# Means of the values of batch 1: eight keys to a row, added on GpSimd, one product on TensorE

## What is computed

```python
B, H, S, D = 2, 8, 768, 64                     # q, k, v are (B, H, S, D), f32
block, window = 32, 16
nb = S // block                                # 24 blocks
k_sum = k.reshape(B, H, nb, block, D).max(axis=3)
v_sum = v.reshape(B, H, nb, block, D).mean(axis=3)
scores_l = q @ k.T / sqrt(D), kept where |pos_q - pos_k| < window
scores_s = q @ k_sum.T / sqrt(D) + log(block)
a = softmax([scores_l, scores_s])              # over both together
attn = a @ [v, v_sum]
x = attn as (B*S, H*D) = (1536, 512)
x = elu(x @ w_in) @ w_out                      # w_in 512x2048, w_out 2048x512
out = gate * (relu(x @ w1[e]) @ w2[e])         # e, gate: best of 8 experts by cosine, per token
```

## Time and profile before

| | |
|---|---|
| three runs | 546.84, 546.86, 547.81 us |
| profiled execution | 546.45 us (span 544.7 us) |
| TensorE (PE) busy | 532.5 us, 98% of the span |
| TensorE weight loads (PEld) | 458.7 us, beside the products |
| VectorE (DVE), ScalarE (ACT), GpSimd (POOL) busy | 301.7, 234.0, 82.0 us |
| granted TensorE clock, mean | 0.998 |

### The profile page before, as it was taken

One profiled execution on the slowest core, in us unless ns is written; L12 is line 12 of the kernel. 1 busy time (PEld: TensorE's weight loads), 2 busy tenths in 40 slices (PEclk: granted clock), 3 DMA queues, 4 the chain that ended last, 5 costly groups with the idle time before them and its releaser, 6 DMA issues.

```text
span 544.7 us, 11801 instructions
## 1 busy us (share of the span) xinstructions
PE 532.5 (98%) x3930; PEld 458.7 (84%) x3931; DVE 301.7 (55%) x667; ACT 234.0 (43%) x530; POOL 82.0 (15%) x210
## 2 busy tenths in 40 slices
PE   8799999999999999999999999999999999999995
PEld 7688888888888888888889898888788888888883
DVE  3789887544644464447542557667583274322552
ACT  5677764443544453444332436461171251211440
POOL 6312020011100000000000000110312131111221
PEclk9999999999999999999999999999999999999999
DMA  9999322232121112110100720010875155101000
GB/s 208 275 273 315 91 48 64 54 75 71 50 64 24 25 25 64 25 25 15 40 1 2 266 84 0 20 59 2 309 256 185 44 206 188 39 28 35 19 19 24
DMA packets 63499, 49.23 MB, mean 90 GB/s; under 512 B 46038, under 2 KB 52182, under 8 KB 63456
## 3 DMA queue, kind: packets, MB, share of 16 engines
q1 hardware_dynamic: 61056, 42.36, 27.1%
q0 software_dynamic: 2400, 6.30, 3.5%
HBM read 43.40 MB, written 6.82 MB: 92 GB/s over the span
## 4 chain that ended last, share of the span: by engine, by line
PE 97%; ACT 1%; issue 1%; DVE 0%; POOLq 0%; DVEq 0%; ACTq 0%
PE bank L976 25%; PE bank L1020 8%; PE bank L1027 8%; PE bank L1033 8%; PE bank L1188 5%; PE bank L1234 5%; PE bank L1242 5%; PE bank L1196 5%; PE bank L1190 5%; PE bank L1236 5%; PE bank L954 3%; PE bank L936 2%; PE bank L927 2%; PE bank L1226 2%; PE bank L1086 1%; PE bank L832 1%
## 5 line engine op out<-in xcount | busy, mean ns | idle before, releaser
L1395 ACT ACTIVATE el<-bank 128x512 f32<-128x512 f32 x48 | 28.7, 597 | 106.0 <-PE bank L976 105.7
L1700 DVE TENSOR_SCALAR el<-el 128x512 f32<-128x512 f32 x48 | 20.7, 431 | 87.8 <-ACT el L1395 87.8
L976 PE MATMUL bank<-x_hi,w_hi_parts 128*128 128x256 f32 x376 | 60.9, 283 | 0.0
L976 PE MATMUL bank<-x_hi,w_lo_parts 128*128 128x256 f32 x376 | 60.4, 282 | 0.0
L976 PE MATMUL bank<-x_lo,w_hi_parts 128*128 128x256 f32 x376 | 60.2, 282 | 0.0
L976 PEld LDWEIGHTS bank<-x_hi,w_hi_parts 128*128 128x128 f32 x376 | 53.6, 188 | 3.2 <-issue 0.2
L1020 PE MATMUL bank<-w_hi_parts,g_hi 128*128 128x512 f32 x192 | 54.9, 408 | 0.0
L1027 PE MATMUL bank<-w_lo_parts,g_hi 128*128 128x512 f32 x192 | 52.8, 397 | 0.0
L1033 PE MATMUL bank<-w_hi_parts,g_lo 128*128 128x512 f32 x192 | 52.5, 395 | 0.0
L976 PEld LDWEIGHTS bank<-x_lo,w_hi_parts 128*128 128x128 f32 x376 | 51.5, 189 | 0.0
L976 PEld LDWEIGHTS bank<-x_hi,w_lo_parts 128*128 128x128 f32 x376 | 51.3, 188 | 0.0
(11 more groups left out here) (282 smaller groups left out, 917.6 us busy)
## 6 DMA issues: line engine op xcount, KB each, us to landing
raw<-in_moe_w SPq DMA_DIRECT2D x8, 2048.0 KB, 8.9
w_raw<-in_moe_w_in SPq DMA_DIRECT2D x8, 512.0 KB, 7.4
w_raw<-in_moe_w_out SPq DMA_DIRECT2D x8, 512.0 KB, 7.6
k_raw<-in_k SPq DMA_DIRECT2D x16, 192.0 KB, 3.2
v_raw<-in_v SPq DMA_DIRECT2D x8, 384.0 KB, 4.3
x_rows<-x SPq DMA_DIRECT2D x6, 512.0 KB, 4.1
q_raw<-in_q SPq DMA_DIRECT2D x44, 64.0 KB, 2.9
vwin<-in_v SPq DMA_DIRECT2D x32, 72.0 KB, 2.8
```

What stands on the lines that cost most here:

```text
L976: mm = pe.matmul(o, r32(w[:, at:at + P]), r32(x[i % 2][:, c, :]), start=(part == "hh" and c == 0), stop=(part == "lh" and c == DC - 1))
L1395: act.activation(el[n % 2], bank[:, H_BANK[n % 2], :], ACT.Exp).then_inc(e_act, 1)
```

## The change

The values of a pair of batch 1 come with eight keys to a partition, on 96 partitions (2048 bytes for each head). GpSimd adds the eight in three additions: four to four, two to two, one to one (512, 256 and 128 elements on each of 96 partitions), each waiting for the one before. TensorE makes one product for the pair, with a new matrix `mean_rows` (96x24) in place of three with `mean`. GpSimd makes `mean_rows` in `means_of_rows`, a memset and two selects of 24 columns, between `constants` and `key_columns(6)`; `means(g)` has one wait more for it (`rows_ok`). `v_raw1` grows from 768 to 1024 columns; `mean`, which only batch 0 still needs, now lies in it ahead of the first load, and `tab` moves from a buffer of its own into scratch space of the attention's zone.

```diff
+    EIGHT = 8
+    V_ROWS = S // EIGHT
...
-        tab = sb("tab", [1, 5, NSTORE], I32)
...
-            {"k_raw1": [P, S], "v_raw1": [P, S], "q_raw0": [P, TB], "q_raw1": [P, TB],
+            {"k_raw1": [P, S], "v_raw1": [P, 2 * EIGHT * D], "q_raw0": [P, TB], "q_raw1": [P, TB],
...
-             "pT": [P, 4 * P], "qT0": [P, TB], "qT1": [P, TB], "mean": [P, KT, NSUM]},
+             "pT": [P, 4 * P], "qT0": [P, TB], "qT1": [P, TB], "mean_rows": [P, NSUM]},
...
+        mean = v_raw1[:, 0:KT * NSUM].rearrange("p (t n) -> p t n", t=KT)
...
+        tab = scratch(1, 5, NSTORE).bitcast(I32)
...
             def load_v1(g):
                 if g > 0:
                     sp.wait_ge(m_mm, PAIRS + g)
-                load_values(H + 2 * g, v_raw1, ld_v1)
+                head = H + 2 * g
+                sp.dma_start(v_raw1[0:V_ROWS, :].rearrange("p (h n) -> p h n", h=2),
+                             vh[head:head + 2].rearrange("h (p t) d -> p h (t d)", p=V_ROWS)).then_inc(ld_v1, 16)
...
+            def means_of_rows():
+                chain(pool.memset(mean_rows[:, :], 1.0 / BLK))
+                chain(pool.affine_select(out=mean_rows, in_=mean_rows, compare_op=ALU.is_ge, fill=0.0, base=0,
+                                         pattern=[[-BLK, NSUM]], channel_multiplier=EIGHT))
+                chain(pool.affine_select(out=mean_rows, in_=mean_rows, compare_op=ALU.is_ge, fill=0.0, base=BLK - 1,
+                                         pattern=[[BLK, NSUM]], channel_multiplier=-EIGHT))
+                pool.sem_inc(rows_ok, 1)
...
             constants()
+            means_of_rows()
             key_columns(6)
...
-            def add_pairs(g):
-
+            def add_eight(g):
+
+                rows = v_raw1[0:V_ROWS, :].rearrange("p (h t d) -> p h t d", h=2, d=D)
                 pool.wait_ge(ld_v1, 16 * g + 16)
-                two = v_raw1.rearrange("p (h t two d) -> p h t two d", h=2, two=2, d=D)
-                pool.tensor_tensor(two[:, :, :, 0, :], two[:, :, :, 0, :], two[:, :, :, 1, :], ALU.add
-                                   ).then_inc(v_two, 1)
+                for n in (4, 2):
+                    chain(pool.tensor_tensor(rows[:, :, 0:n, :], rows[:, :, 0:n, :], rows[:, :, n:2 * n, :], ALU.add))
+                pool.tensor_tensor(rows[:, :, 0, :], rows[:, :, 0, :], rows[:, :, 1, :], ALU.add).then_inc(v_sum, 1)
...
             def means(g):
-                pe.wait_ge(v_two, g + 1)
+                pe.wait_ge(rows_ok, 1)
+                pe.wait_ge(v_sum, g + 1)
                 pe.wait_ge(vs_ev, PAIRS + g)
                 pe.wait_ge(stt, sum(s_at(u) < M_PLACES[g] for u in UNIT_RANGE if u >= PAIRS))
-                src = v_raw1.rearrange("p (h t d) -> p h t d", h=2, d=D)
-                for t in range(0, KT, 2):
-                    mm = pe.matmul(bank[KW:KC, S_BANK[0], 0:P], mean[:, t, :], src[:, :, t, :],
-                                   start=(t == 0), stop=(t == KT - 2))
+                rows = v_raw1[0:V_ROWS, :].rearrange("p (h t d) -> p h t d", h=2, d=D)
+                mm = pe.matmul(bank[KW:KC, S_BANK[0], 0:P], mean_rows[0:V_ROWS, :], rows[:, :, 0, :],
+                               start=True, stop=True)
                 mm.then_inc(m_mm, 1)
```

More of the change, by code:

```diff
@@ L261, in build @@
         W_HI = W_HI[:, :]
-        (k_raw1, v_raw1, q_raw0, q_raw1, vwin, kT, kb0, kb1, kmaxT, mask, pr0, pr1, pT, qT0, qT1, mean,
+        (k_raw1, v_raw1, q_raw0, q_raw1, vwin, kT, kb0, kb1, kmaxT, mask, pr0, pr1, pT, qT0, qT1, mean_rows,
          raw, c_sb, iota_m) = zone(
             "att",
-            {"k_raw1": [P, S], "v_raw1": [P, S], "q_raw0": [P, TB], "q_raw1": [P, TB],
+            {"k_raw1": [P, S], "v_raw1": [P, 2 * EIGHT * D], "q_raw0": [P, TB], "q_raw1": [P, TB],
              "vwin": [P, PAIRS, WINS, P], "kT": [P, PAIRS, KPAD], "kb0": [P, WINS, KC], "kb1": [P, WINS, KC],
              "kmaxT": [P, PAIRS, NSUM], "mask": [P, 3, KC], "pr0": [P, 4, KC], "pr1": [P, 4, KC],
-             "pT": [P, 4 * P], "qT0": [P, TB], "qT1": [P, TB], "mean": [P, KT, NSUM]},
+             "pT": [P, 4 * P], "qT0": [P, TB], "qT1": [P, TB], "mean_rows": [P, NSUM]},
             {"raw": [P, WSZ], "c_sb": [P, 1536], "iota_m": [P, P]})
+        mean = v_raw1[:, 0:KT * NSUM].rearrange("p (t n) -> p t n", t=KT)
         q_raw, qT, kb = (q_raw0, q_raw1), (qT0, qT1), (kb0, kb1)
@@ L342, in build @@
         ld_win, ld_wout = (sems(" ".join(f"{a}_{s}" for s in range(STEPS))) for a in ("ld_win", "ld_wout"))
-        vw_zero, ident_ok, pads_ok, mean_ok, mask_ok, const_ok, iota_ok, xs_zero = sems(
-            "vw_zero ident_ok pads_ok mean_ok mask_ok const_ok iota_ok xs_zero")
+        vw_zero, ident_ok, pads_ok, mean_ok, rows_ok, mask_ok, const_ok, iota_ok, xs_zero = sems(
+            "vw_zero ident_ok pads_ok mean_ok rows_ok mask_ok const_ok iota_ok xs_zero")
         dve_c, pool_c, passed = sems("dve_c pool_c passed")
-        k_t, k_ev, kmx, kb_ev, q_t, q_ev, v_two, m_mm, vs_ev = sems(
-            "k_t k_ev kmx kb_ev q_t q_ev v_two m_mm vs_ev")
+        k_t, k_ev, kmx, kb_ev, q_t, q_ev, v_sum, m_mm, vs_ev = sems(
+            "k_t k_ev kmx kb_ev q_t q_ev v_sum m_mm vs_ev")
         s_mm, mask_h, mask_l, unit_ok, stt, smax, expd, rden_v, rinv_v, norm_v, p_t, pT_ev, o_mm, xh_ev, xl_ev = sems(
@@ L730, in _ @@
             key_columns(8)
-            def add_pairs(g):
+            def add_eight(g):
+                rows = v_raw1[0:V_ROWS, :].rearrange("p (h t d) -> p h t d", h=2, d=D)
                 pool.wait_ge(ld_v1, 16 * g + 16)
-                two = v_raw1.rearrange("p (h t two d) -> p h t two d", h=2, two=2, d=D)
-                pool.tensor_tensor(two[:, :, :, 0, :], two[:, :, :, 0, :], two[:, :, :, 1, :], ALU.add
-                                   ).then_inc(v_two, 1)
+                for n in (4, 2):
+                    chain(pool.tensor_tensor(rows[:, :, 0:n, :], rows[:, :, 0:n, :], rows[:, :, n:2 * n, :], ALU.add))
+                pool.tensor_tensor(rows[:, :, 0, :], rows[:, :, 0, :], rows[:, :, 1, :], ALU.add).then_inc(v_sum, 1)
             for u in range(9, UNITS):
                 if 0 <= u - 3 * PAIRS < PAIRS:
-                    add_pairs(u - 3 * PAIRS)
+                    add_eight(u - 3 * PAIRS)
                 key_columns(u)
```

## The result

The changed kernel takes 542.39 us (median of four runs, 542.21 to 543.25) against 547.3 us before (546.84 to 547.81): ratio 0.9908, 95% interval [0.9896, 0.9921]. The profiled execution took 542.21 us, with a span of 540.5 us.

A forecast was written before the change was run, and what follows sets the result against it. TensorE, busy 98% of the span, was taken to bound the kernel. Sixteen records fewer save 1.76 us, all other terms count as nothing: 546.86 - 1.76 = 545.1 us, range 544.5 to 546.7 us.

The forecast's parts named there:

- What bounds the kernel: TensorE, busy 98% of the span, sets the end; time taken off its queue comes off the end.
- the three waits behind 160 us: TensorE's waits after all four means, 0.4 to 0.6 us each, 1.3 us together, expected to move with TensorE.
- What is removed on TensorE: At batch 1's means, four records fewer per pair at 0.11 us: 0.44 us a pair, 1.76 us for four.
- the 0.12 us of the change of shape and the idle 0.20 us: Part of each means piece that stays, ending with the weight side idle for 0.20 us behind the means.
- The cheap record of batch 0: Rival price from batch 0's means: 0.060 us a record, 0.95 us saved, 545.9 us; chance of its family 0.18.
- the 55.6 ns of the Trainium skill: Rival price from the skill's page for successive 128-column products: 16 records at 55.6 ns, 0.89 us saved.
- The wait for `rows_ok`: One wait more per pair in TensorE's queue at the means: taken at nothing, at most 0.8 us in all.
- What is added to GpSimd: A pair's additions take 2.5 us, bounds 1.93 and 3.03, so 1.5 us more, all off the path.
- the cover: Slack hiding longer GpSimd additions: sums over 8 us early; delayed VectorE instructions end by 81.8 us, read from 83.21.
- The profiled execution and the median: The median of three runs was put 0.41 us above the profiled execution, giving 546.86 us before the change.
- Buffers: Large buffers slide by 560 bytes, those behind by 16; an address was taken to have no price.
- Rivals: Records worth less, 0.18; gain taken back behind, 0.09; GpSimd late, 0.05; change not doing what it says, part of 0.09.

The follow-up runs named there:

- e9: The changed kernel with the weights 32 bytes lower and the buffers of x, g and h 32 bytes higher; 535.91 us.
- e7: The changed kernel with two 32-byte buffers allocated behind the attention's zone, so that the weights begin at 21440; 535.98 us, ratio 0.9789.
- e10: The kernel before, its work untouched, with the weights 64 bytes lower and the buffers of x, g and h 32 bytes higher; 536.32 us, ratio 0.9797.
- e1: The kernel before again, unchanged, for a second trace; 547.75 us.
- e5: The kernel before with `tab` moved into scratch space and 32 bytes left free, weights at 21504 as in the changed kernel; 543.68 us, ratio 0.9935.
- e3: The changed kernel with `gate_cur` allocated behind the attention's zone, so that the weights begin 32 bytes lower; 544.45 us, ratio 0.9942.
- e8: The changed kernel with the buffers of x, g and h 64 bytes higher and the weights where they are; 533.92 us, ratio 0.9753.

## Why the prediction was right and wrong

- **What bounds the kernel:** right. The 1.75 us and the unforeseen gains of TensorE reached the end, but for e9 and e7, where later loads ahead of the means took up most of the 1.75 us (0.4 and 0.3 us left against e10). One reading was off: the shortest of the three waits behind 160 us is 0.3 us, not 0.4; their sum of 1.3 us holds.
- **What is removed on TensorE:** right. 0.44 us for a pair forecast, 0.435 to 0.444 measured; the 0.12 us of the change of shape and the idle 0.20 us stayed. The cheap record of batch 0 (0.060 us, 0.95 us in all) and the 55.6 ns of the Trainium skill (TensorE: Matmul & The Clock Gate, "Wait — 56ns, not 53.3ns?"; 0.89 us, measured with bf16) both fail as prices of these f32 records by the steps: a removed record gave back 0.11 us. The 96 partitions cost nothing.
- **The wait for `rows_ok`:** costs nothing that the 0.33 us piece would show.
- **What is added to GpSimd:** 2.6 us for a pair (2.09 + 0.46) where 2.5 was taken, and the sums stood at 116.5 us for a product at 124.95, 8.5 us early (8.7 forecast). The first pair's took 3.8 us, beyond the 3.0 us of the bound, since VectorE was busy beside it; its two instructions there took 1.03 and 1.75 us in place of 0.69 and 1.22. VectorE's two ended at 80.4 us, and their readers start at 82.71 us and later, so the cover held. The contention that the Trainium skill names (GPSIMD Engine Reference, "1. Specifications") is in this trace; its rule against additions on GpSimd ("4.1 Engine selection") would have misled on the time.
- **The profiled execution and the median:** wrong by a little. The median had been put 0.41 us above the profiled execution; over 17 runs beside the first experiments it was 547.5 us, 1.05 us above. The profiled execution lacked part of the early waits that e1 shows, 1.1 us by 60 us. The changed kernel's profiled execution lies only 0.18 us below its median. Its loads of `w_in` land sooner (5.9 in place of 7.4 us); that this is why is not shown.
- **Buffers:** this is the step that failed. It said that the buffers slide and that "an address has no price that the trace could show", on the ground of three forms of L976 with 283, 282 and 282 ns. Twice wrong. The duration of a record holds its way through the array and hides 1 or 2 ns of pace: the same three forms have 284, 282 and 282 ns in the changed kernel. The distance between starts, or the length of 24 in the chain, shows it. And the three forms could not have told: `w_hi_parts` and `w_lo_parts` lie 65536 bytes apart, `x_hi0` and `x_lo0` 4096, and each tile within them starts a multiple of 512 bytes further. All of them have one and the same distance up to a multiple of 512. The comparison held the disputed quantity fixed. The slide itself was mis-sized too: 480 bytes in place of 560, and 64 bytes up in place of 16 down for the buffers behind. Measured in e5, the moved `tab` and the slid buffers are worth 3.8 us, over twice the work that the change is named for.
- **Rivals:** none of the four happened. Unnamed costs of moved buffers were put on the slower side alone; they were a gain, and twice the size of the forecast.

The forecast direction was right for its reason, and the size was wrong for a cause that the change carries along. That this cause helped and did not hurt was luck: the forecast had no term for it, and other slides of 32 or 64 bytes made the changed kernel 2.1 us slower (e3) or 6 to 8 us faster (e7, e8). A line that moves a table of 480 bytes did more than the new way of the means.

## What to carry to other kernels

Where a kernel is bound by long runs of products and an edit changes any buffer's size or place, compare the pace of untouched products (starts, not durations) before the gain is put down to the edit; one run with the same work and a pad of 32 or 64 bytes tells the two apart. Here a pad of 64 bytes in one place, with no instruction changed, took 8.5 us off the changed kernel and made the fastest kernel of all that were tried (533.9 us, ratio to before 0.9753 [0.9738, 0.9768]). To argue that a quantity has no price, take rows between which it varies.

## What was not expected of the hardware

- The pace of TensorE's products follows the distance between the buffers of their two factors, up to a multiple of 512 bytes (or of 256, which no run tells apart): 114.6 to 119.7 ns for 256 columns and 229.1 to 233.7 ns for 512, all at a granted clock of 0.996 to 0.999. The Trainium skill (SBUF — State Buffer, "A bandwidth-pool intuition that's wrong (but worth ruling out)") gives TensorE a second, independent read port for its weights. That the pace hangs on a distance between the two speaks against two reads that never meet, if it is the reads that meet. That was not tried, and why 448 (x or g minus weights) is fast for both shapes while 0 is fast for 512 columns alone stays open. Seven of the sixteen distances that are multiples of 32 were tried.
- Loads of 512 KB in 1024-byte pieces landed in 5.9 to 6.3 us (medians) where their buffer begins at a multiple of 512, and in 6.9 to 7.7 us elsewhere.
- GpSimd's three additions, 2.6 us alone, took 3.8 us beside two instructions of VectorE with two inputs, which took 1.5 and 1.4 times as long themselves.
